# Attention and two mixtures of experts on one core: the gate normalization on VectorE cut into three shares per round

## What is computed

```python
def _moe2_ref(x, w_gate, w1, w2):      # N, D = 2304, 512; E = 8; F = 1024
    logits = x @ w_gate
    logits = logits - logits.max()
    P = np.exp(logits)
    for _ in range(8):
        P /= P.sum(1, keepdims=True) + 1e-09
        P /= P.sum(0, keepdims=True) + 1e-09
        P *= N / E
    out = np.zeros((N, D), dtype=np.float32)
    for e in range(E):
        h = np.maximum(x @ w1[e], 0.0)
        ye = h @ w2[e]
        out += P[:, e:e + 1] * ye
    return out.astype(np.float32)
```

## Time and profile before

| | us |
|---|---|
| median of 3 runs | 977.72 |
| the profiled execution | 976.18 |
| its span in the profile | 974.4 |
| PE busy (9740 matmuls) | 950.7 (98%) |
| VectorE busy | 727.9 (75%) |
| POOL busy | 616.9 (63%) |
| ACT busy | 563.2 (58%) |

### The profile page before, as it was taken

One profiled execution on the slowest core, in us unless ns is written; L12 is line 12 of the kernel. 1 busy time (PEld: TensorE's weight loads), 2 busy tenths in 40 slices (PEclk: granted clock), 3 DMA queues, 4 the chain that ended last, 5 costly groups with the idle time before them and its releaser, 6 DMA issues.

```text
span 974.4 us, 25643 instructions
## 1 busy us (share of the span) xinstructions
PE 950.7 (98%) x9740; PEld 891.5 (91%) x9740; DVE 727.9 (75%) x2023; ACT 563.2 (58%) x1370; POOL 616.9 (63%) x563
## 2 busy tenths in 40 slices
PE   6999999899999999999999999999999999999998
PEld 4778665599999999999999999999999999999998
DVE  6777756488886787678767876787678767876775
ACT  5777623445576666556655665566556655665542
POOL 5555420245877497749774977497749784978453
PEclk9999999999999999999999999999999999999999
DMA  5788779602002200220022002200220022001111
GB/s 205 249 292 294 265 286 401 248 2 88 1 2 88 87 1 2 88 88 2 1 88 87 2 1 88 88 2 1 87 88 2 1 87 88 1 1 44 44 45 65
DMA packets 36953, 87.70 MB, mean 90 GB/s; under 512 B 3041, under 2 KB 3041, under 8 KB 36833
## 3 DMA queue, kind: packets, MB, share of 16 engines
q1 hardware_dynamic: 36832, 86.07, 24.3%
HBM read 81.35 MB, written 4.72 MB: 88 GB/s over the span
## 4 chain that ended last, share of the span: by engine, by line
PE 85%; DVE 7%; ACT 4%; issue 3%; DMA 1%; SPq 0%; POOL 0%; DVEq 0%; ACTq 0%; POOLq 0%
PE bank L974 22%; PE bank L976 21%; PE bank L978 21%; PE bank L934 7%; PE bank L862 2%; PE bank L652 2%; ACT scores L1039 2%; PE bank L700 1%; PE bank L917 1%; PE bank L641 1%; DMA raw<-big_w_in 1%; DVE acc L1572 1%; PE bank L685 1%; DVE s_sum L1500 1%; DVE s_sum L1488 1%
## 5 line engine op out<-in xcount | busy, mean ns | idle before, releaser
L569 POOL TENSOR_TENSOR s_split<-s_sum,s_split 128x512 fp32r<-128x512 f32 x288 | 367.7, 1296 | 190.2 <-ACT s_split L1123 187.5
L1572 DVE SCALAR_TENSOR_TENSOR acc<-bank,gate_now,acc 128x256 f32<-128x256 f32 x441 | 222.5, 515 | 147.6 <-PE bank L978 146.8
L1123 ACT ACTIVATE s_split<-s_sum 128x512 fp32r<-128x512 f32 x288 | 181.5, 632 | 253.8 <-DVE s_sum L1483 138.3
L974 PE MATMUL bank<-t_split,s_split 128*128 128x256 f32 x1008 | 281.0, 279 | 3.2 <-DVE acc L1572 3.0
L976 PE MATMUL bank<-t_split,s_split 128*128 128x256 f32 x1008 | 279.0, 277 | 0.0
L978 PE MATMUL bank<-t_split,s_split 128*128 128x256 f32 x1008 | 279.0, 277 | 0.0
L974 PEld LDWEIGHTS bank<-t_split,s_split 128*128 128x128 f32 x1008 | 189.3, 188 | 7.9 <-DVE acc L1572 4.2
L978 PEld LDWEIGHTS bank<-t_split,s_split 128*128 128x128 f32 x1008 | 189.7, 188 | 0.0
L976 PEld LDWEIGHTS bank<-t_split,s_split 128*128 128x128 f32 x1008 | 189.3, 188 | 0.0
L974 PE MATMUL bank<-t_split,a 128*128 128x256 f32 x576 | 161.0, 279 | 0.3 <-DVE acc L1566 0.3
L976 PE MATMUL bank<-t_split,a 128*128 128x256 f32 x576 | 159.6, 277 | 0.0
(11 more groups left out here) (224 smaller groups left out, 1972.0 us busy)
## 6 DMA issues: line engine op xcount, KB each, us to landing
raw<-big_w_in SPq DMA_DIRECT2D x14, 2048.0 KB, 8.2
mid_raw<-slot_w_in SPq DMA_DIRECT2D x8, 1024.0 KB, 8.7
early_raw<-slot_w_in SPq DMA_DIRECT2D x8, 1024.0 KB, 9.9
ring_raw<-slot_w_in SPq DMA_DIRECT2D x7, 1024.0 KB, 6.0
late_raw<-slot_w_in SPq DMA_DIRECT2D x6, 1024.0 KB, 9.4
q_ring<-q_tiles SPq DMA_DIRECT2D x18, 256.0 KB, 5.7
k_ring<-k_tiles SPq DMA_DIRECT2D x18, 256.0 KB, 5.3
out_rows<-acc SPq DMA_DIRECT2D x18, 256.0 KB, 2.0
```

The costliest lines, as they stand in the source:

```text
L569: pool.tensor_tensor(s_split[:, i, 1, :, :], s_sum[:, i, :, :], s_split[:, i, 0, :, :].bitcast(F32), ALU.subtract)\
L974: pe.matmul(to, left[:, 0, f, :], t_place(parity, k, 0)[:, f, :], start=(f == 0 and k in FRESH), stop=False, skip_group_check=k not in FRESH)
L1123: act.activation(s_split[:, i, 0, :, :], s_sum[:, i, :, :], ACT.Copy).then_inc(s_hi_ready, 1)
L1572: done = dve.scalar_tensor_tensor(out=to, in0=got, scalar=gate, in1=to, op0=ALU.mult, op1=ALU.add)
```

## The change

Each round is cut into three shares at three successive products: after product n only the reciprocal is taken before the addition, and the scaling by it comes behind the addition and the sums of that product; the row sums and their reciprocal come at the end of product n+1; the scaling by rows and the column sums at the end of product n+2. The rounds move to other products, 4 to 7 apart. Both reciprocals are now kept in SBUF (`gate_stat[:, 1]`, `row_stat[:, 1]`).

```diff
-    GATES_AT, MAX_AT, SHARE_AT, EXP_AT = (0, 1), (0, 2), (0, 4), (1, 0)
-    ROUND_AT = [(1, 4), (2, 1), (2, 4), (3, 2), (4, 0), (5, 0), (6, 0), (7, 0)]
+    GATES_AT, MAX_AT, SHARE_AT, ROWS_AT_FIRST = (0, 1), (0, 2), (0, 4), (1, 1)
+    ROUND_AT = [(2, 0), (2, 4), (3, 2), (4, 0), (4, 4), (5, 2), (6, 0), (7, 0)]
+    ROWS_SLOTS = [PRODUCTS * p + k for p, k in [ROWS_AT_FIRST]] + [PRODUCTS * p + k + 1 for p, k in ROUND_AT[:-1]]
+    assert all(b - a >= 3 for a, b in zip(ROWS_SLOTS, [PRODUCTS * p + k for p, k in ROUND_AT]))
...
-                ("gates", [P, TILES + 1, GATES + 1]), ("row_stat", [P, TILES]), ("gate_stat", [P, GATES]),
+                ("gates", [P, TILES + 1, GATES + 1]), ("row_stat", [P, 2, TILES]), ("gate_stat", [P, 2, GATES]),
...
-            def rows_then_columns(small):
-                link(dve.tensor_reduce(row_stat[:, :], gates[:, 0:TILES, :], AX.X, ALU.add))
-                inv = small[:, 2 * P + 2 * GATES:2 * P + 2 * GATES + TILES]
-                link(dve.reciprocal(inv, row_stat[:, :]))
-                link(dve.tensor_tensor(kept, kept, inv.unsqueeze(2).to_broadcast([P, TILES, GATES]), ALU.mult))
-                dve.tensor_reduce(gate_stat[:, 0:GATES], gates[:, :, 0:GATES].rearrange("p t g -> p g t"), AX.X, ALU.add)\
-                   .then_inc(gate_vec, 1)
...
                 if (p, k) in ROUND_AT:
-                    inv = small[:, 2 * P + GATES:2 * P + 2 * GATES]
-                    link(dve.reciprocal(inv, small[:, 2 * P:2 * P + GATES]))
-                    scaled = dve.scalar_tensor_tensor(out=kept, in0=kept, scalar=float(N) / EXPERTS,
-                                                      in1=inv.unsqueeze(1).to_broadcast([P, TILES, GATES]), op0=ALU.mult, op1=ALU.mult)
-                    if (p, k) == ROUND_AT[-1]:
-                        scaled.then_inc(gate_vec, 1)
-                        dve.wait_ge(gate_vec, 5 + SINKHORN_ROUNDS)
-                    else:
-                        link(scaled)
-                        rows_then_columns(small)
+                    link(dve.reciprocal(gate_stat[:, 1, :], small[:, 2 * P:2 * P + GATES]))
+                if (p, k) == ROUND_AT[-1]:
+                    scale_columns().then_inc(gate_vec, 1)
+                    dve.wait_ge(gate_vec, 5 + SINKHORN_ROUNDS)
+
+            def scale_columns():
+                return dve.scalar_tensor_tensor(out=kept, in0=kept, scalar=float(N) / EXPERTS,
+                                                in1=gate_stat[:, 1, :].unsqueeze(1).to_broadcast([P, TILES, GATES]), op0=ALU.mult, op1=ALU.mult)
+
+            def gate_share(p, at):
+                n = PRODUCTS * p + at
+                if (p, at) in ROUND_AT[:-1]:
+                    link(scale_columns())
+                if n in ROWS_SLOTS:
+                    if n == ROWS_SLOTS[0]:
+                        dve.wait_ge(gate_act, 1)
+                    link(dve.tensor_reduce(row_stat[:, 0, :], gates[:, 0:TILES, :], AX.X, ALU.add))
+                    link(dve.reciprocal(row_stat[:, 1, :], row_stat[:, 0, :]))
+                if n - 1 in ROWS_SLOTS:
+                    link(dve.tensor_tensor(kept, kept, row_stat[:, 1, :].unsqueeze(2).to_broadcast([P, TILES, GATES]), ALU.mult))
+                    dve.tensor_reduce(gate_stat[:, 0, :], gates[:, :, 0:GATES].rearrange("p t g -> p g t"), AX.X, ALU.add)\
+                       .then_inc(gate_vec, 1)
...
                         if ahead and at - late in (1, 3):
                             sums_second(n1, (parity1 + p1) % 2, (at - late) // 2, before)
+                        if first:
+                            gate_share(p, at)
```

More of the change, by code:

```diff
@@ L134, in attention_then_two_moes @@
     PHASE = 112
-    GATES_AT, MAX_AT, SHARE_AT, EXP_AT = (0, 1), (0, 2), (0, 4), (1, 0)
-    ROUND_AT = [(1, 4), (2, 1), (2, 4), (3, 2), (4, 0), (5, 0), (6, 0), (7, 0)]
-    assert all(k in FRESH for _, k in [GATES_AT, MAX_AT, SHARE_AT, EXP_AT] + ROUND_AT)
+    GATES_AT, MAX_AT, SHARE_AT, ROWS_AT_FIRST = (0, 1), (0, 2), (0, 4), (1, 1)
+    ROUND_AT = [(2, 0), (2, 4), (3, 2), (4, 0), (4, 4), (5, 2), (6, 0), (7, 0)]
+    assert all(k in FRESH for _, k in [GATES_AT, MAX_AT, SHARE_AT] + ROUND_AT)
+    ROWS_SLOTS = [PRODUCTS * p + k for p, k in [ROWS_AT_FIRST]] + [PRODUCTS * p + k + 1 for p, k in ROUND_AT[:-1]]
+    assert all(b - a >= 3 for a, b in zip(ROWS_SLOTS, [PRODUCTS * p + k for p, k in ROUND_AT]))
     assert len(ROUND_AT) == SINKHORN_ROUNDS
@@ L949, in gate_step @@
                     pe.wait_ge(gate_vec, 5 + ROUND_AT.index((p, k)))
-                    pe.matmul(to[:, 2 * P:2 * P + GATES], ones[:, :], gate_stat[:, 0:GATES], start=True, stop=True)
+                    pe.matmul(to[:, 2 * P:2 * P + GATES], ones[:, :], gate_stat[:, 0, :], start=True, stop=True)
             def product(e, p, at, k, parity, first):
@@ L1526, in gate_step @@
                     dve.tensor_scalar(one_stat[:, 2:3], small[:, 2 * P:2 * P + 1], -1.0, None, ALU.mult).then_inc(gate_vec, 1)
-                if (p, k) == EXP_AT:
-                    dve.wait_ge(gate_act, 1)
-                    rows_then_columns(small)
                 if (p, k) in ROUND_AT:
-                    inv = small[:, 2 * P + GATES:2 * P + 2 * GATES]
-                    link(dve.reciprocal(inv, small[:, 2 * P:2 * P + GATES]))
-                    scaled = dve.scalar_tensor_tensor(out=kept, in0=kept, scalar=float(N) / EXPERTS,
-                                                      in1=inv.unsqueeze(1).to_broadcast([P, TILES, GATES]), op0=ALU.mult, op1=ALU.mult)
-                    if (p, k) == ROUND_AT[-1]:
-                        scaled.then_inc(gate_vec, 1)
-                        dve.wait_ge(gate_vec, 5 + SINKHORN_ROUNDS)
-                    else:
-                        link(scaled)
-                        rows_then_columns(small)
+                    link(dve.reciprocal(gate_stat[:, 1, :], small[:, 2 * P:2 * P + GATES]))
[18 more added lines that the diff above has]
+                       .then_inc(gate_vec, 1)
             def targets(p, k):
```

## The result

The changed kernel takes 992.55 us in the median of 4 runs (991.12 to 993.04), the kernel before, on the same chips, 977.15; the ratio is 1.0158, with an interval of 1.0136 to 1.0180. It is slower, as forecast, but by 15.4 us instead of 9.4, and the time lies above the range (991.0). The profiled execution took 991.12 us, span 989.0, 14.6 more than before.

A forecast was written before the change was run, and what follows sets the result against it. PE was taken to bound the kernel. With held scalings, pair lengths summed to 89.95 us against 80.54, +9.4; 976.18 + 9.4 = 985.6 for the profiled execution, given as 986, range 978.5 to 991.

The forecast's parts named there:

- the wait at (4, 4): Pair 4, product 4: PE waits for column sums from the round four products earlier; 2.8 us, or 5.8 with held scalings.
- The bound on a gain: Pairs 1 to 7 could at best take 77.6 us, so the change can win at most 2.9 us, 0.3%.
- PE as the bound: Whole kernel: PE bounds it; pairs 1 to 7 take 80.54 us, a product 1.36 us.
- The hold: Scalings with two SBUF inputs wait until POOL's running instruction ends; +9.4 us in pairs 1 to 7, chance 0.48.
- races won: Rival: scalings wait for POOL, but VectorE starts first where margins are 0.1 us; +4.4 us, chance 0.18.
- no hold: Rival: two-input scalings don't wait for POOL, only the column-sum wait costs; +1.8 us, 978.0 us, chance 0.20.
- not slower: Rival: PE doesn't wait at pair 4, product 4; -1.8 us, 974.4 us, chance 0.06.
- a heavier hold: Rival: blocked VectorE also lets POOL's next instruction pass, or SBUF reciprocals are held too; +14 us and more, chance 0.08.
- Pair 4: Fourth pair of expert 0: 13.75 us without scalings held by POOL, 17.3 us with them.
- Held, adds 0.5: End of pair 3: the third share of round (3, 2), held by POOL, adds 0.5 us to pair 4.
- Pair 6: Sixth pair: 11.3 us without held scalings; 13.1 with them, the column scaling waiting 0.8 us and the third share 1.2.
- Pairs 1, 2, 3, 5: With scalings held by POOL, these pairs take 11.75, 14.9, 11.05 and 10.75 us.

The follow-up runs named there:

- before_sbuf: The kernel before the change, with only both reciprocals kept in SBUF: 982.78 us, ratio 1.0055 to the kernel before.
- ahead_sbuf: The changed kernel with the first and third shares' work ahead of their product's add, row reciprocal in the third share, reciprocals in SBUF: 978.76 us, ratio 1.0021.
- warm_wait: The changed kernel plus 20 identity matmuls on PE ahead of its wait at pair 4, product 4: 991.82 us, ratio 1.0151 to the kernel before.
- ahead_psum: The changed kernel with the first and third shares' work ahead of their product's add, row reciprocal in the third share, reciprocals in PSUM: 975.67 us, ratio 0.9994.
- rounds_at_4: The kernel before, whole rounds and PSUM reciprocals kept, most rounds moved to product 4: 973.56 us, ratio 0.9965; measured again, 974.96 us, 0.9977.
- after_no44: The changed kernel with seven rounds instead of eight, the one at pair 4, product 4 left out: 988.12 us, ratio 1.0107 to the kernel before.

## Why the prediction was right in kind and short in size

By the earlier trace rows the forecast's pairs come to 89.9 us and measured 95.8. The step that failed is the price of the wait at (4, 4): the sum has the wait and nothing for PE's clock behind it, which fell to 0.50 and cost 2.0 us. Of the other 3.9, about 1.5 come from third shares that make PE start pairs 4 and 6 late (below), and about 1.2 from scalings in pairs 6 and 7 that met another instruction of POOL than forecast. Besides, 986 is 1 us low by its own working: 977.72 + 9.4 is 987.1.

- **The bound on a gain, and PE as the bound:** right. The best version found, at 78.4 us in pairs 1 to 7, stays over the 77.6 worked out.
- **The hold:** right, and now shown for the case that no row of before had, a VectorE instruction with two SBUF inputs as the loser. It ends 0.16 to 0.17 behind POOL's end (246.27 and 246.11; 251.21 and 251.04), each of the twelve held ones within 0.16 to 0.18. The races went as forecast: POOL was first by 0.11 in pair 4, so *races won* falls; *no hold* falls by before_sbuf and ahead_sbuf; *not slower* by the 5.65 us wait.
- **The rival by size,** a heavier hold at +14 and more, had the number, not the mechanism: the reciprocals in SBUF are free (266 ns, also under POOL's instruction at 247.99), and each held scaling ends with the first POOL instruction that it met.
- **Pair 4, forecast 17.3, was 20.0: the step that failed most.** The wait at (4, 4) was 5.8 in the forecast and 5.65 in the trace. What the forecast left out is what 5.65 us of idleness does to PE: the granted clock fell (0.50 for the 4.0 us behind the wait; matmuls of 0.41 where they take 0.28), 2.0 us by warm_wait. The 5.8 stood in the forecast and the clock of the kernel before was read at 1.00; I didn't ask what it would be behind such a gap. Most of the other 0.7 is a later start of (4, 0), below.
- **"Held, adds 0.5"** for the third share of round (3, 2), and none for that of (5, 2): mis-sized, and with it the premise that a share is there in time where the next round is 5 to 7 products on: (4, 0) and (6, 0) are 5 on, and PE waits 0.8 us at each. In pair 6 PE starts its gate matmul 1.92 us into the pair, not 0.96, and in pair 4 1.93: 1.0 us each. The third L571 of POOL in the pair before begins at 11.0 on its clock, ahead of the share at 11.5.
- **Pair 6, 13.1 forecast, 14.8 measured:** besides that 1.0, the column scaling came at 5.9 on the pair's clock and not at 4.8, because PE's wait moves VectorE's work, while POOL's weight work stands 0.8 earlier on this clock than before. So the scaling met the *next* weight instruction and was held to 7.4 instead of 5.6. In the same way the last scaling, in pair 7, which I left unchanged, met one and took 1.87 us: 11.63 from 11.07. The places of POOL's work on a pair's clock were read in a trace in which the pairs had other lengths.
- **Pairs 1, 2, 3, 5:** 11.85, 15.26, 11.14, 11.14 against 11.75, 14.9, 11.05, 10.75: right to 0.4.
- **What the 15.3 us are made of.** Shown: 2.0 are the clock, and 4.6, these 2.0 among them, go with the round at (4, 4) (20.01 less 15.43). The hold costs 5.6 in whole rounds and 2.6 with shares ahead of the add. In the change's own order it wasn't measured by itself. By the forecast, +1.8 would be left without it, and the one wait of ahead_psum agrees with the forecast's times; so I put some 11.5 us down to the hold and 2 to the clock behind the wait that it lengthened. That split is argued, not shown.

The Trainium skill, "SBUF — State Buffer", section "Who interferes with whom", gives this rule: a VectorE instruction with two SBUF inputs contends with a GpSimd instruction that reads SBUF, and whichever is issued later is blocked until the earlier is over. The traces agree in each kernel here with SBUF scratch, up to 2.24 us for an instruction of 0.30.

## What to carry to other kernels

Before a small operand is moved from PSUM to SBUF, count the SBUF inputs of the VectorE instructions that read it and look at what POOL runs then: an instruction of 0.3 us took 2.2 here. Cutting a serial piece of work into shares shortens each stop but puts off its result; take the consumer's due time from the trace and check the last share against it, and where a wait of some microseconds on TensorE comes out, add what the clock will cost behind it. Here it was better to leave the piece whole and put it where its engine has two products with nothing but an add behind (rounds_at_4, 0.2 to 0.35% faster).

## What I hadn't expected of the hardware

- 5.65 us without a matmul in a dense stretch were followed by 4.0 us at a granted clock of 0.50, with matmuls of 0.41 us for 0.28; 20 small matmuls in the gap removed it all. In after_no44, where PE is held in pieces of up to 1.7 us, the pairs' clock stays at 1.00.
- PE has two paces at full clock, 1.36 and 1.41 us a product. Pair 5 of rounds_at_4 has the slow one (11.07 us); in the second profile of the same kernel it has the fast one (10.70). So the instructions alone don't set it, and what does remains open.
